# An attention and mixture-of-experts kernel on one core: order of x, maxima and first weights, and where sinks' rows and clearings are done

## The chip, the cores and the metric

One NeuronCore of a Trainium2 chip runs the whole program. The metric is the device time of one execution in microseconds. The kernel before takes 1252.02 us, the median of three runs (1251.76, 1252.02, 1252.05).

## The reference

Three layers follow one another. The change touches the first of them and the loads of weights for the second.

```python
# attention: q, k, v are (2, 8, 768, 64), n_sink = 4, window = 128
scores = scale * np.matmul(q, k.transpose(0, 1, 3, 2))
keep = is_sink | in_window            # keys 0..3, or 0 <= query - key < 128
scores = np.where(keep, scores, -1000000000.0)
a = np.exp(scores - scores.max(-1)) ; a = a / (a.sum(-1) + 1e-09)
x = (a @ v), heads side by side       # 1536 x 512
# SoLU layer: w_in (512, 1024), w_out (1024, 512)
h = x @ w_in ; solu = h * softmax(h) ; x = layernorm(solu) * g_ln @ w_out
# eight experts, every token through each
P = exp(x @ w_gate - max), 8 rounds of scaling rows and columns
out = sum over e of P[:, e] * (relu(x @ w1[e]) @ w2[e])
```

## The kernel before, in words

**Stages.** The program is written engine by engine; each engine runs its own list in order, and semaphores join them. The attention stage takes the first 93.88 us, then comes the SoLU layer (`h1_half` and what follows), then the experts. Where a product needs more than fp32r gives, both of its factors are split into a rounded part and a rest, and three products are summed (L797 to L799). So x, w_in, w_out and the sinks' rows of v each exist as a rounded part ("round_", "hi") and a rest ("rest_"), made by different instructions.

**Attention.** `PAIRS` is 8: a pair is two heads, side by side on the partitions (64 rows each). A head has `QT` = 6 tiles of 128 queries. A tile of queries sees its own 128 keys, the 128 before, and the 4 sinks, so its scores are 128, 256 or 260 columns wide. The probabilities at the sinks are handled apart, as `sink_cols`, since the rows of v at the sinks (`v_sink`, 72 partitions: a rounded copy at row 0, a second at row 32, the rest at row 64, each with 4 rows for either head) meet all tiles in one product.

**TensorE** goes through a pair as scores(p,1), back(p,0), scores(p,2), back(p,1), and so on up to scores(p+1,0), back(p,5). Scores (L722) lie in four banks, so the product for a tile waits until VectorE and ScalarE have read the one two tiles earlier. `back` does the rest of older tiles, three batches of two tiles to a pair: back(p,0) transposes batch 1 of pair p-1 (L742), back(p,1) multiplies its batch 0 by v (L766), back(p,2) transposes batch 2, back(p,3) transposes `sink_cols` (L750) and multiplies batch 1, back(p,4) transposes batch 0 of pair p itself, back(p,5) multiplies batch 2 and the sinks' rows (L773), which completes x of pair p-1. The first scores of a pair wait for its q and k (`qk_loaded`).

**VectorE** takes each tile from its bank, adds the mask and finds the row maximum in one instruction (`mask_max`, L1270). Between tiles its `back` normalises a batch (sum and reciprocal, L1278 and L1282, then the probabilities of one head, L1285), makes the rest of x (`rest_x`, L1303), copies transposed probabilities to SBUF (`copy_pT`, L1291) and makes the rest of v's sink rows (`rest_v_sinks`, L1297).

**ScalarE** takes the exponentials of each tile (L1042), scales probabilities (L1057), copies transposed ones (L1049, L1061) and rounds x of a pair (`round_x`, L1066), which frees the bank of x for the next pair together with `rest_x`.

**GpSimd** clears tensors and builds the masks (L481 to L509), and then in each pair: `normalise(p,0)` for the other head (L517), `rest_w_in` (L565), `normalise(p,1)`, `lay_sinks(p+1)` (L550: copies the sinks' columns of k beside each block), `rest_w_out` (L571), `normalise(p,2)`, `split_sinks` (L540, L543), `round_v_sinks` (L527), `round_segments(p+1)` (L556, L559). The weights of the SoLU layer come in eight segments, one for a pair, each 128x512 of w_in and of w_out, all through one buffer, `w_raw`. In pair 0 the order differs: normalise(0,0), normalise(0,1), lay_sinks(1), round_segments(0), rest_w_in(0), rest_w_out(0), normalise(0,2), and on.

**SyncE** issues all loads, in the order of its list. After q, k of pairs 0 and 1 it waits for the cleared `v_sink`, loads v of pair 0 (L400) with six little transfers of 4x64 into `v_sink` (L403), segment 0 (L408, L409), two small tensors and v of pair 1. Then comes the loop, whose order is: q and k of pair p, v of pair p-1, then segment p as soon as the rests of segment p-1 are made:

```python
for p in range(1, PAIRS):
    if p >= 2:
        sp.wait_ge(scores_full, STEPS * (p - 1))
        load_qk(p)
    if p >= 3:
        sp.wait_ge(x_full, p - 2)
        for h in range(2): load_v(p - 1, h)
    sp.wait_ge(in_done, p)      # rest_w_in(p - 1) is made
    sp.wait_ge(out_done, p)     # rest_w_out(p - 1) is made
    load_segments(p)
```

So q and k of pair 2 are issued behind segment 1, and this behind `rest_w_out(0)` (L571).

## Time and profile before

| | before |
|---|---|
| median of 3 runs | 1252.02 us |
| profiled execution | 1253.09 us |
| its span in the trace | 1251.3 us |
| TensorE busy | 1236.2 us, 99% |
| VectorE busy | 691.7 us, 55% |
| GpSimd busy | 535.7 us, 43% |
| ScalarE busy | 365.1 us, 29% |
| TensorE's share of the chain that ended last | 95% |

The span is the time from the first to the last instruction that the profiler recorded; the execution's own time is 1.8 us longer. Busy shares are means over the whole span, so they say little of the first 94 us, in which all four engines work side by side; a window over that stage alone has to be read for it. Timelines give the start of each instruction, its length, and in brackets the idle time of its engine before it with the work that ended it.

### The profile page before, as it was taken

How to read it: one execution, taken by the hardware profiler on the slowest of the kernel's cores; microseconds unless marked ns; L12 is line 12 of the kernel's file. 1: busy time of each engine (PE TensorE's matmuls, PEld its weight loads, DVE VectorE, ACT ScalarE, POOL GpSimd, SP SyncE). 2: the span in 40 equal slices, each digit the busy share in tenths (PEclk: the TensorE clock that was granted, in tenths of full speed). 3: DMA queues.
4: the chain of work that ended last, by engine and by line, in shares of the span. 5: the costliest groups of instructions: out<-in, count | busy, mean ns of one | idle time of the engine just before them, and what ended most of it. 6: DMA issues, size and time to landing. Idle time of an engine off the chain costs nothing.

```text
span 1251.3 us, 18785 instructions
## 1 busy us (share of the span) xinstructions
PE 1236.2 (99%) x6446; PEld 1097.3 (88%) x6446; DVE 691.7 (55%) x1348; ACT 365.1 (29%) x832; POOL 535.7 (43%) x625
## 2 busy tenths in 40 slices
PE   7999999999999999999999999999999999999998
PEld 4558899989988999999999999999999999999997
DVE  7895734356665555555555555555555555555554
ACT  7884634312233222222222222222222222222221
POOL 7772315644444444444444444444444444444440
PEclk9999999999999999999999999999999999999999
DMA  6440000111110111111111111111111111111102
GB/s 204 156 149 18 1 1 1 34 35 34 34 35 28 38 36 36 34 34 34 34 34 34 34 34 34 34 34 34 34 34 34 34 34 34 34 34 34 35 18 101
DMA packets 57264, 53.13 MB, mean 42 GB/s; under 512 B 4352, under 2 KB 44544, under 8 KB 57216
## 3 DMA queue, kind: packets, MB, share of 16 engines
q1 hardware_dynamic: 56928, 52.19, 13.1%
q8 instruction: 27, 0.44, 0.1%
q10 hardware_dynamic: 288, 0.33, 0.1%
q14 instruction: 21, 0.17, 0.0%
HBM read 49.35 MB, written 3.15 MB: 42 GB/s over the span
## 4 chain that ended last, share of the span: by engine, by line
PE 95%; ACT 2%; DVE 2%; DMA 1%; issue 1%; SPq 0%; DVEq 0%; ACTq 0%
PE ps L797 30%; PE ps L798 30%; PE ps L799 30%; PE ps L722 2%; PE ps L766 1%; PE ps L742 1%; PE ps L847 1%; ACT probs L1042 1%; ACT acc L1218 1%; DVE probs L1270 1%; DMA k_sb<-kT 0%; PE ps L977 0%; DVE xw L1303 0%; ACT xw L1066 0%; DMA q_sb<-qT 0%
## 5 line engine op out<-in xcount | busy, mean ns | idle before, releaser
L1528 DVE SCALAR_TENSOR_TENSOR acc<-ps,gate_now,acc 128x512 f32<-128x512 f32 x336 | 252.1, 750 | 166.2 <-PE ps L799 162.0
L797 PE MATMUL ps<-ring 128*128 128x512 f32 x768 | 300.6, 391 | 0.0
L798 PE MATMUL ps<-ring 128*128 128x512 f32 x768 | 299.8, 390 | 0.0
L799 PE MATMUL ps<-ring 128*128 128x512 f32 x768 | 299.2, 390 | 0.0
L1200 ACT ACTIVATE sums<-ps 128x384 f32<-128x384 f32 x192 | 94.4, 492 | 597.8 <-PE ps L799 597.8
L1504 DVE TENSOR_TENSOR sums<-ps,sums 128x384 f32<-128x384 f32 x192 | 106.9, 557 | 158.2 <-ACT sums L1200 106.9
L799 PEld LDWEIGHTS ps<-ring 128*128 128x128 f32 x768 | 144.3, 188 | 30.9
L797 PEld LDWEIGHTS ps<-ring 128*128 128x128 f32 x768 | 144.2, 188 | 27.9 <-DVE acc L1524 0.4
L798 PEld LDWEIGHTS ps<-ring 128*128 128x128 f32 x768 | 144.2, 188 | 25.8
L642 POOL TENSOR_TENSOR w_raw<-w_raw 128x256 f32<-128x256 f32 x32 | 23.7, 741 | 321.3 <-PE ps L799 321.3
L797 PE MATMUL ps<-xw,ring 128*128 128x384 f32 x448 | 152.5, 340 | 0.3 <-ACT sums L1200 0.2
L1510 DVE SCALAR_TENSOR_TENSOR ring<-sums,ring 128x384 fp32r<-128x384 f32 x192 | 112.0, 583 | 72.9 <-ACT ring L1211 72.9
L799 PE MATMUL ps<-xw,ring 128*128 128x384 f32 x448 | 151.0, 337 | 0.0
L798 PE MATMUL ps<-xw,ring 128*128 128x384 f32 x448 | 150.9, 337 | 0.0
L797 PE MATMUL ps<-xw,w_b 128*128 128x384 f32 x448 | 150.5, 336 | 0.0
L799 PE MATMUL ps<-xw,w_b 128*128 128x384 f32 x448 | 150.3, 336 | 0.0
L798 PE MATMUL ps<-xw,w_b 128*128 128x384 f32 x448 | 150.0, 335 | 0.0
L671 POOL TENSOR_SCALAR ring<-w_in 128x1024 fp32r<-128x1024 f32 x32 | 33.8, 1056 | 233.0 <-PE ps L799 178.2
L1211 ACT ACTIVATE ring<-sums 128x384 fp32r<-128x384 f32 x192 | 100.1, 521 | 85.7 <-DVE sums L1504 85.7
L797 PEld LDWEIGHTS ps<-xw,ring 128*128 128x128 f32 x448 | 84.1, 188 | 2.6 <-ACT sums L1200 0.5
L798 PEld LDWEIGHTS ps<-xw,w_b 128*128 128x128 f32 x448 | 84.3, 188 | 2.0
L797 PEld LDWEIGHTS ps<-xw,w_b 128*128 128x128 f32 x448 | 84.1, 188 | 1.9
(148 smaller groups left out, 1765.2 us busy)
## 6 DMA issues: line engine op xcount, KB each, us to landing
w_in<-w_exp SPq DMA_DIRECT2D x64, 256.0 KB, 3.2
w_raw<-w_exp SPq DMA_DIRECT2D x64, 128.0 KB, 2.8
w_raw<-w_exp SPq DMA_DIRECT2D x32, 256.0 KB, 3.2
v_sb<-v SPq DMA_DIRECT2D x16, 192.0 KB
out<-acc SPq DMA_DIRECT2D x12, 256.0 KB, 2.0
q_sb<-qT SPq DMA_DIRECT2D x7, 384.0 KB, 4.4
k_sb<-kT SPq DMA_DIRECT2D x7, 384.0 KB, 4.9
k_sb<-kT SPq DMA_DIRECT2D x9, 256.0 KB, 5.7
```

Of the source, the lines that this page charges most:

```text
L642: pool.tensor_tensor(raw(4), raw(0), raw(3), ALU.add).then_inc(w1_sums, 1)
L671: pool.tensor_scalar(w2c(0, 0, 2 * BANK), w2_raw(0, 2 * BANK), 1.0, 0.0, ALU.mult, ALU.add).then_inc(w2_hi, 1)
L722: pe.matmul(bank(k % S_BANKS)[:, 0:w], q_sb[rows_h, p % 2, t * P:(t + 1) * P], k_sb[rows_h, p % 2, k_at(t), at:at + w], start=True, stop=T ...
L742: last = pe.transpose(t_bank(p, use)[:, at:at + P], p_block(p, h, n), ident[:, :])
L797: pe.matmul(o, ws[0], xs[0], start=first, stop=False, skip_group_check=True)
L798: pe.matmul(o, ws[0], xs[1], start=False, stop=False, skip_group_check=True)
L799: return pe.matmul(o, ws[1], xs[0], start=False, stop=last, skip_group_check=True)
L1200: act.activation(part_sum(m, s), a_bank(s), ACT.Copy).then_inc(part_copied, 1)
L1211: act.activation(h_at(0, i, b * BLK, BLK), a_bank(s) if m == C12 else c_sum(m), ACT.Relu).then_inc(h_hi_out, 1)
L1504: dve.tensor_tensor(c_sum(m), at, part_sum(part, s), ALU.add).then_inc(c_summed, 1)
L1510: dve.scalar_tensor_tensor(out=h_at(1, i, b * BLK, BLK), in0=a_bank(s) if m == C12 else c_sum(m), scalar=0.0, in1=h_at(0, i, b * BLK, BLK) ...
L1528: dve.scalar_tensor_tensor(out=acc[:, T, :], in0=y_bank(u, T), scalar=gate_now[:, T:T + 1], in1=acc[:, T, :], op0=ALU.mult, op1=ALU.add).t ...
```

## The change

It has four parts, all in the attention stage.

1. **x first, maxima ahead.** On ScalarE `round_x(p-2)` stands ahead of the exponentials of pair p's first tile, and `scale_probs(p-1, 2)` moves from tile 0 to tile 1. On VectorE what stood between the masks of tile 0 and tile 1 (normalise(p-1,2), rest_x, copy_pT) now stands behind the masks of tile 1, with rest_x as the first of it.
2. **Sinks' rows of v in four parts.** All pairs' rows are loaded at the start by six transfers of 4x8x64, issued behind segment 0, in place of 48 of 4x64. GpSimd makes the rounded part and the rest for two pairs at once, in pairs 0, 2, 4 and 6; VectorE's L1297 is gone.
3. **Clearing by VectorE.** `v_sink` (now 72x1024), `sink_cols`, `wg` and `ones` are cleared or set by VectorE ahead of its first work, no longer by GpSimd.
4. **First weights.** In pair 0 GpSimd runs normalise(0,0), round_segments(0), normalise(0,1), lay_sinks(1), rest_w_in(0), normalise(0,2), split_sinks(0), rest_w_out(0), split_v_sinks(0), round_segments(1).

```diff
@@ sync
             def load_v(p, h):
                 sp.dma_start(v_sb[:, p % 2, h, :], v[p, h]).then_inc(v_loaded[p % 2], 16)
+            def load_v_sinks(h):
                 for row in (0, 32, 64):
                     row += h * NS
-                    sp.dma_start(v_sink[row:row + NS, p % 2, h * DH:(h + 1) * DH],
-                                 v[p, h, 0:NS, 0:DH]).then_inc(v_loaded[p % 2], 16)
+                    sp.dma_start(v_sink[row:row + NS, :, h * DH:(h + 1) * DH],
+                                 v[:, h, 0:NS, 0:DH].rearrange("p n d -> n p d")).then_inc(v_sinks_loaded, 16)
...
             load_qk(1)
-            sp.wait_ge(consts, 2)
             for h in range(2):
                 load_v(0, h)
             load_segments(0)
+            sp.wait_ge(v_sinks_clear, 1)
+            for h in range(2):
+                load_v_sinks(h)
...
@@ gpsimd
-            pool.memset(v_sink[:, :], 0.0).then_inc(consts, 1)
...
-            pool.memset(sink_cols[:, :, :].bitcast(F32), 0.0).then_inc(sinks_hi, 1)
...
-            pool.memset(ones[:, :], 1.0).then_inc(consts, 1)
-            pool.memset(wg[:, :, :].bitcast(F32), 0.0).then_inc(consts, 1)
...
+            def split_v_sinks(p):
+                two = slice(p, p + 2)
...
+                pool.tensor_scalar(v_sink_r[:, two, :], v_sink[:, two, :], 1.0, 0.0,
                                    ALU.mult, ALU.add).then_inc(v_sinks_hi, 1)
...
+                low = v_sink_r[64:SINK_ROWS, two, :]
+                pool.tensor_tensor(low, v_sink[64:SINK_ROWS, two, :], low.bitcast(F32),
+                                   ALU.subtract).then_inc(v_sinks_split, 1)
...
             for p in range(PAIRS):
                 normalise(p, 0)
-                if p > 0:
+                if p == 0:
+                    round_segments(0)
+                else:
                     rest_w_in(p)
                 normalise(p, 1)
                 if p + 1 < PAIRS:
                     lay_sinks(p + 1)
                 if p == 0:
-                    round_segments(0)
                     rest_w_in(0)
-                rest_w_out(p)
+                else:
+                    rest_w_out(p)
                 if p == 4:
                     rest_router()
                 normalise(p, 2)
                 split_sinks(p)
-                round_v_sinks(p)
+                if p == 0:
+                    rest_w_out(0)
+                if p % 2 == 0:
+                    split_v_sinks(p)
                 if p + 1 < PAIRS:
                     round_segments(p + 1)
@@ scalar
-                if t == 0 and p > 1:
-                    round_x(p - 2)
                 if t == 0 and p > 0:
                     copy_pT(p - 1, 1, 0)
+                if t == 1 and p > 0:
                     scale_probs(p - 1, 2)
...
             for p in range(PAIRS):
+                if p > 1:
+                    round_x(p - 2)
                 for t in range(QT):
@@ vector
-                if t == 0 and p > 0:
-                    normalise(p - 1, 2)
+                if t == 1 and p > 0:
                     if p > 1:
                         rest_x(p - 2)
+                    normalise(p - 1, 2)
                     copy_pT(p - 1, 1, 1)
...
-                if t == 3 and p > 0:
-                    rest_v_sinks(p - 1)
...
+            dve.memset(v_sink[:, :, :], 0.0).then_inc(v_sinks_clear, 1)
+            dve.memset(sink_cols[:, :, :].bitcast(F32), 0.0).then_inc(sink_cols_clear, 1)
+            dve.memset(wg[:, :, :].bitcast(F32), 0.0).then_inc(router_clear, 1)
+            dve.memset(ones[:, :], 1.0).then_inc(ones_set, 1)
```

GpSimd's list in pair 0, before:

```order
L517 TENSOR_TENSOR probs<-probs,a_stat 128x256
L517 TENSOR_TENSOR probs<-probs,a_stat 128x260 x2
L550 TENSOR_SCALAR k_sb<-k_sb 128x5x4 x2
L556 TENSOR_SCALAR xw<-w_raw 128x512
L559 TENSOR_SCALAR w_end<-w_raw 128x512
L565 TENSOR_TENSOR xw<-w_raw,xw 128x512
L571 TENSOR_TENSOR w_end<-w_raw,w_end 128x512
L517 TENSOR_TENSOR probs<-probs,a_stat 128x260 x2
L540 TENSOR_SCALAR sink_cols<-probs 128x4x8 x2
L543 TENSOR_TENSOR sink_cols<-probs,sink_cols 128x4x8
L527 TENSOR_SCALAR v_sink_r<-v_sink 72x128
```

and in the changed kernel, where lines are numbered anew (normalise L519, roundings L564 and L567, lay_sinks L558, rests L573 and L579):

```order
L519 TENSOR_TENSOR probs<-probs,a_stat 128x256
L564 TENSOR_SCALAR xw<-w_raw 128x512
L567 TENSOR_SCALAR w_end<-w_raw 128x512
L519 TENSOR_TENSOR probs<-probs,a_stat 128x260 x2
L558 TENSOR_SCALAR k_sb<-k_sb 128x5x4 x2
L573 TENSOR_TENSOR xw<-w_raw,xw 128x512
L519 TENSOR_TENSOR probs<-probs,a_stat 128x260 x2
L548 TENSOR_SCALAR sink_cols<-probs 128x4x8 x2
L551 TENSOR_TENSOR sink_cols<-probs,sink_cols 128x4x8
L579 TENSOR_TENSOR w_end<-w_raw,w_end 128x512
L528 TENSOR_SCALAR v_sink_r<-v_sink 72x256
L532 TENSOR_TENSOR v_sink_r<-v_sink,v_sink_r 8x256
```

Both roundings moved ahead of normalise(0,1), and the last instruction that SyncE's loop waits for (L571, now L579) moved behind normalise(0,2) and split_sinks.

VectorE's list where pair 1 passes into pair 2, before:

```order
L1270 ISA probs,a_stat<-ps,mask 128x128
L1270 ISA a_stat 128x1
L1278 TENSOR_SCALAR a_stat<-a_stat 128x4
L1282 RECIPROCAL a_stat<-a_stat 128x4
L1285 TENSOR_SCALAR probs<-probs,a_stat 128x260
L1303 TENSOR_TENSOR xw<-ps,xw 128x768
L1291 COPY pT<-ps 128x512
L1270 ISA probs,a_stat<-ps,mask 128x256
L1270 ISA a_stat 128x1
```

and in the changed kernel (masks L1287, normalise L1295 to L1302, copy L1308, rest_x L1314):

```order
L1287 ISA probs,a_stat<-ps,mask 128x128
L1287 ISA a_stat 128x1
L1287 ISA probs,a_stat<-ps,mask 128x256
L1287 ISA a_stat 128x1
L1287 ISA probs,a_stat<-ps,mask 128x256
L1287 ISA a_stat 128x1
L1314 TENSOR_TENSOR xw<-ps,xw 128x768
L1295 TENSOR_SCALAR a_stat<-a_stat 128x4
L1299 RECIPROCAL a_stat<-a_stat 128x4
L1302 TENSOR_SCALAR probs<-probs,a_stat 128x260
L1308 COPY pT<-ps 128x512
```

The masks of both heads of tile 1 (128x256) moved ahead of the other four steps, and rest_x ahead of normalise.

SyncE's list from the loads of v of pair 0 on, before:

```order
L400 DMA v_sb<-v 128x384
L403 DMA v_sink<-v 4x64 x3
L400 DMA v_sb<-v 128x384
L403 DMA v_sink<-v 4x64 x3
L408 DMA w_raw<-w_in 128x512
L409 DMA w_raw<-w_out 128x512
```

and in the changed kernel:

```order
L402 DMA v_sb<-v 128x384 x2
L412 DMA w_raw<-w_in 128x512
L413 DMA w_raw<-w_out 128x512
L407 DMA v_sink<-v 4x8x64 x6
L427 DMA g_col<-g_ln 128x8
L428 DMA wg_raw<-w_gate 128x32
```

The segment is now issued ahead of all transfers to `v_sink`; the loop behind it keeps its order.

## Rows read from the trace of the kernel before

**Rows 1.** Windows: length, busy us of PE, PEld, DVE, ACT, POOL, clock, DMA share, GB/s.

```profile
3.00:11.00 8.00, 6.89 (x34) 4.77 (x34) 5.76 (x29) 5.60 (x22) 4.41 (x13) 1.00 1.06 359
23.70:80.65 56.95, 53.58 (x395) 33.71 (x395) 50.72 (x187) 48.21 (x159) 42.30 (x83) 1.00 0.53 175
93.88:1251.30 1157.42, 1153.95 (x5863) 1045.34 (x5863) 612.31 (x1049) 288.71 (x583) 465.73 (x483) 1.00 0.10 32
```

**Rows 2.** Timeline of TensorE at pair 2: start, length, what, idle before it.

```profile
23.72 0.49 PE L722 MATMUL ps<-k_sb,q_sb 64*128 64x128 f32 x4 [1.27 <-DMA k_sb<-kT]
```

**Rows 3.** Timeline of the DMA queue of SyncE: start, issue time.

```profile
7.19 0.35 SPq L408 DMA_DIRECT2D w_raw<-w_in  x1
...
15.56 0.35 SPq L408 DMA_DIRECT2D w_raw<-w_in  x1
```

**Rows 4.** Chain of waits, pair 2: start, length.

```profile
17.95 5.72 DMA k_sb<-kT
```

**Rows 5.** DMA issues up to 9 us: count, size, us to landing.

```profile
w_raw<-w_in SPq DMA_DIRECT2D x1, 256.0 KB, 4.0
```

**Rows 6.** Issue times in ns of one DMA line: minimum/median/maximum.

```profile
L409 SPq DMA_DIRECT2D w_raw<-w_out x3: 432/433/892, 7.6 to 26.3; - x3
```

**Rows 7.** Timeline of GpSimd in pair 0.

```profile
10.25 1.25 POOL L517 TENSOR_TENSOR probs<-probs,a_stat 128x260 f32<-128x260 f32 x2 [1.22 <-DVE a_stat L1282]
11.47 0.38 POOL L550 TENSOR_SCALAR k_sb<-k_sb 128x20 f32<-128x20 f32 x2
...
12.97 1.27 POOL L565 TENSOR_TENSOR xw<-w_raw,xw 128x512 fp32r<-128x512 f32 x1
14.20 1.27 POOL L571 TENSOR_TENSOR w_end<-w_raw,w_end 128x512 fp32r<-128x512 f32 x1
15.43 1.25 POOL L517 TENSOR_TENSOR probs<-probs,a_stat 128x260 f32<-128x260 f32 x2
16.87 0.40 POOL L540 TENSOR_SCALAR sink_cols<-probs 128x32 fp32r<-128x32 f32 x2 [0.19 <-POOL probs L517]
...
17.57 0.30 POOL L527 TENSOR_SCALAR v_sink_r<-v_sink 72x128 fp32r<-72x128 f32 x1
```

**Rows 8.** Timeline of VectorE at the start and in pair 1.

```profile
3.96 0.56 DVE L1328 COPY k_sb<-k_sb 128x20 f32<-128x20 f32 x2 [3.11 <-DMA q_sb<-qT]
...
21.57 0.42 DVE L1285 TENSOR_SCALAR probs<-probs,a_stat 128x260 f32<-128x260 f32 x1
```

**Rows 9.** Timeline of VectorE, pair 4 (begun at 46.19).

```profile
48.69 0.17 DVE L1278 TENSOR_SCALAR a_stat<-a_stat 128x4 f32<-128x4 f32 x1 [0.40 <-ACT probs L1042]
...
49.11 0.82 DVE L1285 TENSOR_SCALAR probs<-probs,a_stat 128x260 f32<-128x260 f32 x1
50.15 0.96 DVE L1303 TENSOR_TENSOR xw<-ps,xw 128x768 fp32r<-128x768 f32 x1 [0.23 <-ACT xw L1066]
51.03 0.68 DVE L1291 COPY pT<-ps 128x512 f32<-128x512 f32 x1
51.62 0.41 DVE L1270 CUSTOM_DVE_ANT_0 probs<-ps,mask 128x256 f32<-128x256 f32 x1
...
55.62 0.50 DVE L1297 TENSOR_TENSOR v_sink_r<-v_sink,v_sink_r 8x128 fp32r<-8x128 f32 x1
```

**Rows 10.** Timeline of GpSimd, pair 4.

```profile
49.15 1.25 POOL L517 TENSOR_TENSOR probs<-probs,a_stat 128x260 f32<-128x260 f32 x2 [0.38 <-DVE a_stat L1282]
```

**Rows 11.** Timeline of ScalarE, pair 4.

```profile
52.08 0.51 ACT L1042 ACTIVATE probs<-probs,a_stat 128x256 f32<-128x256 f32 x1 [1.08 <-DVE a_stat L1270]
...
54.07 0.57 ACT L1049 ACTIVATE pT<-ps 128x512 f32<-128x512 f32 x1
```

**Rows 12.** Timeline of TensorE, pairs 4 and 5.

```profile
54.79 0.60 PE L750 MATMUL ps<-ident,sink_cols 128*72 128x128 f32 x4
...
57.57 0.49 PE L722 MATMUL ps<-k_sb,q_sb 64*128 64x128 f32 x4
...
59.66 0.70 PE L722 MATMUL ps<-k_sb,q_sb 64*128 64x256 f32 x4
```

More of the change, by code:

```diff
@@ L121, in solu_moe @@
         SINK_ROWS = 64 + 2 * NS
-        v_sink = sb("v_sink", [SINK_ROWS, 2, P], F32, in_a)
-        v_sink_r = sb("v_sink_r", [SINK_ROWS, 2, P], F32R, in_a)
+        v_sink = sb("v_sink", [SINK_ROWS, PAIRS, P], F32, in_a)
+        v_sink_r = sb("v_sink_r", [SINK_ROWS, PAIRS, P], F32R, in_a)
         sink_cols = sb("sink_cols", [P, QT - 2, SINK_ROWS], F32R, in_a)
@@ L219, in solu_moe @@
         sinks_hi, sinks_split = sem("sinks_hi"), sem("sinks_split")
+        sink_cols_clear, router_clear, ones_set = sem("sink_cols_clear"), sem("router_clear"), sem("ones_set")
+        v_sinks_clear, v_sinks_loaded = sem("v_sinks_clear"), sem("v_sinks_loaded")
         v_sinks_hi, v_sinks_split = sem("v_sinks_hi"), sem("v_sinks_split")
@@ L519, in normalise @@
                 last.then_inc(probs_ready[1], 1)
-            def round_v_sinks(p):
-                pool.wait_ge(v_loaded[p % 2], 128 * (p // 2 + 1))
-                if p >= 2:
-                    pool.wait_ge(x_full, p - 1)
+            def split_v_sinks(p):
+                two = slice(p, p + 2)
                 if p == 0:
-                    pool.wait_ge(consts, 2)
-                pool.tensor_scalar(v_sink_r[:, p % 2, :], v_sink[:, p % 2, :], 1.0, 0.0,
+                    pool.wait_ge(v_sinks_loaded, 96)
+                pool.tensor_scalar(v_sink_r[:, two, :], v_sink[:, two, :], 1.0, 0.0,
                                    ALU.mult, ALU.add).then_inc(v_sinks_hi, 1)
+                pool.wait_ge(v_sinks_hi, p // 2 + 1)
+                low = v_sink_r[64:SINK_ROWS, two, :]
+                pool.tensor_tensor(low, v_sink[64:SINK_ROWS, two, :], low.bitcast(F32),
+                                   ALU.subtract).then_inc(v_sinks_split, 1)
+                pool.wait_ge(v_sinks_split, p // 2 + 1)
             def split_sinks(p):
@@ L534, in split_sinks @@
                     pool.wait_ge(probs_ready[h], BATCHES * (p + 1))
-                if p > 0:
+                if p == 0:
+                    pool.wait_ge(sink_cols_clear, 1)
+                else:
                     pool.wait_ge(pT_full, T_USES * (p - 1) + SINK_USE + 1)
@@ L541, in split_sinks @@
                 last.then_inc(sinks_hi, 1)
-                pool.wait_ge(sinks_hi, p + 2)
+                pool.wait_ge(sinks_hi, p + 1)
                 pool.tensor_tensor(sink_cols[:, :, 32:32 + n], a, sink_cols[:, :, 0:n].bitcast(F32),
@@ L581, in _ @@
                 normalise(p, 0)
-                if p > 0:
+                if p == 0:
+                    round_segments(0)
+                else:
                     rest_w_in(p)
@@ L587, in _ @@
                 if p == 0:
-                    round_segments(0)
                     rest_w_in(0)
-                rest_w_out(p)
+                else:
+                    rest_w_out(p)
                 if p == 4:
@@ L594, in _ @@
                 split_sinks(p)
-                round_v_sinks(p)
+                if p == 0:
+                    rest_w_out(0)
+                if p % 2 == 0:
+                    split_v_sinks(p)
                 if p + 1 < PAIRS:
@@ L758, in pv @@
                 if b == 0:
-                    pe.wait_ge(v_loaded[p % 2], 128 * (p // 2 + 1))
+                    pe.wait_ge(v_loaded[p % 2], 32 * (p // 2 + 1))
                     if p > 0:
@@ L771, in pv_sinks @@
                 pe.wait_ge(*copied(p, SINK_USE))
-                pe.wait_ge(v_sinks_split, p + 1)
-                pe.matmul(x_psum(2, QT), v_sink_r[:, p % 2, :], sinkT[:, :],
+                pe.wait_ge(v_sinks_split, p // 2 + 1)
+                pe.matmul(x_psum(2, QT), v_sink_r[:, p, :], sinkT[:, :],
                           start=False, stop=True, skip_group_check=True).then_inc(x_full, 1)
@@ L788, in back @@
                     if p == 0:
-                        pe.wait_ge(consts, 3)
+                        pe.wait_ge(consts, 2)
                     turn(p, 0)
@@ L990, in gate_step @@
                 if step == "logits":
+                    pe.wait_ge(ones_set, 1)
                     gate_logits()
@@ L1091, in _ @@
                     act.wait_ge(small_loaded, 32)
-                    act.wait_ge(consts, 5)
+                    act.wait_ge(router_clear, 1)
                     act.activation(wg[:, :, WG_AT:WG_AT + EXPERTS], wg_raw[:, :, :], ACT.Copy).then_inc(wg_ready, 1)
@@ L1155, in tile @@
                 turned_pair(T + 1, 1)
+            round_x(PAIRS - 2)
             back(PAIRS, 0)
+            back(PAIRS, 1)
             exp_h(0)
@@ L1335, in _ @@
                     back(p, t)
-            back(PAIRS, 0)
+            back(PAIRS, 1)
             TURNED = {4: (0, 0), 5: (0, 4), 7: (1, 0), 8: (1, 4), 10: (2, 0), 11: (2, 4)}
@@ L1403, in _ @@
             copy_pT(PAIRS - 1, 2, 1)
-            rest_v_sinks(PAIRS - 1)
             solu(1)
```

7 lines of the change are left out of this document (1 added, 6 removed).

## Prediction

> **What bounds the kernel now.** I read the windows first, because the change touches only the attention stage. From 93.88 us to the end TensorE is busy 1153.95 of 1157.42 us, at the full clock (1.00), and VectorE and GpSimd are busy for about half and two fifths of it [rows 1]. Nothing there waits for what the change moves, so that stretch keeps its length, and whatever the attention stage gains or loses goes to the end one for one. The stage before it is 93.88 us, 7.5% of the kernel.
>
> Inside it the windows show a different picture. From 23.70 to 80.65 us five pairs of heads pass, 56.95 us or 11.39 us for each; PE is busy 53.58 us, DVE 50.72, ACT 48.21 and POOL 42.30 [rows 1]. No engine is full, so a loop of waits through several engines sets the period. The timelines of pair 4 give its steps [rows 9 to 12].
>
> The start is bound by something else. The timeline of TensorE shows that the scores of pair 2 began at 23.72 us after 1.27 us of idleness that a load of k ended [rows 2], and the chain of waits goes through that same load, issued at 17.95 and 5.72 us long [rows 4]. Its issue is late because SyncE's queue runs in order: the weights of the next segment are issued ahead of it, at 15.56 [rows 3], and they wait until GpSimd has finished the rest of the first w_out segment (L571), which ended when the next instruction began, at 15.43 [rows 7].
>
> **The change part by part.**
>
> *First weights, another order on GpSimd.* Before, pair 0 ran: normalise(0,1), lay_sinks, two roundings, rest_w_in, rest_w_out, normalise(0,2), split_sinks. Now the roundings stand ahead of normalise(0,1), and rest_w_out stands behind split_sinks. Two things follow.
>
> First, the roundings wait for the weights. These were issued at 7.19 us [rows 3] and landed 4.0 us later [rows 5], at 11.2. They are now issued sooner, since the six little v transfers that stood ahead come behind them, but from 3 to 11 us the DMA share was 1.06 [rows 1]: the engines were full of q, k and v loads, so I leave the landing at 11.2. GpSimd was free to begin normalise(0,1) at 10.25 [rows 7]; now it stands behind the wait.
>
> Second, the end of rest_w_out moves. From the timeline of GpSimd [rows 7]: normalise took 11.47 - 10.25 = 1.22 us, lay_sinks and both roundings 12.97 - 11.47 = 1.50, rest_w_in 1.23, rest_w_out 1.23, normalise(0,2) with split_sinks 17.57 - 15.43 = 2.14. The new order from the landing: 11.2 + 1.22 + 1.50 + 1.23 + 2.14 + 1.23 = 18.5 us, where 15.43 stood. SyncE's queue, which waits for exactly this, is **3.1 us later**: the weights of segment 1, and behind them q and k of pair 2. From the issue of the weights to the landing of k it took 17.95 + 5.72 - 15.56 = 8.1 us. Within it one issue took 0.89 us where the median of its line is 0.43 [rows 6], so 7.6 is possible. k for pair 2 then lands between 18.6 + 7.6 = 26.2 and 18.65 + 8.1 = 26.8, against 23.7: TensorE was 1.27 us idle there already, so all of it counts. I take **+2.8 us**, bounds +2.5 and +3.1. The pieces of work that are moved cost the same; what costs is that a queue stands behind the last one.
>
> *x first, and the maxima of tile 1 ahead.* On ScalarE round_x of the pair before last stands ahead of the exponentials of tile 0. On VectorE the masks of tile 1 (L1270) come before rest_x (L1303), and normalise(p-1,2) behind it. Before, VectorE idled 0.40 us for exponentials and 0.23 for round_x [rows 9], and ScalarE 1.08 us for the masks of tile 1 [rows 11]. These waits go, and the loop closes elsewhere: TensorE issues scores(p,1) behind the last products with v, so the masks of tile 1 wait for it. I add the new loop once round. TensorE from the transposed sinks to the scores of the next pair, 57.57 - 54.79 = 2.78; on to scores of tile 1, 59.66 - 57.57 = 2.09; until these are complete 0.70 [rows 12]. VectorE: two masks, 0.41 each less the 0.07 by which neighbours overlap, 0.69; rest_x, 51.03 - 50.15 = 0.88; normalise, 49.11 - 48.69 = 0.42 and 0.82 less 0.08, 1.16; copy, 0.59 [rows 9]. Then the mask of tile 2 to its exponential, 52.08 - 51.62 = 0.46 [rows 9, 11]; two exponentials, half of 54.07 - 52.08, 1.00; the copy that frees the bank and TensorE's start behind it, 54.79 - 54.07 = 0.72 [rows 11, 12]. Sum 11.07 us, against 11.39: 0.32 less per pair. Over five pairs and the last interval up to 93.88 that is 1.9 us. It is a sum without chance holds, which the measured 11.39 contains, and so I count half: **-1.0 us**, bounds 0 and -1.9.
>
> One step of this sum rests on a hold. VectorE's L1285 took 0.82 us in pair 4 and 0.42 in pair 1 [rows 8, 9]; in pair 4 GpSimd had begun its own normalise 0.04 us after it [rows 10] and VectorE ended well behind GpSimd's first instruction. The same two are released together in the new order, so 0.82 stays in my sum. The Trainium skill (SBUF — State Buffer, section Who interferes with whom) says that whoever issues first of a two-port VectorE instruction and a GpSimd one gets the shared pair of ports for the whole instruction. By that rule VectorE, which began first, would not have been held. The row differs, and the row decides; by the rule the period would be some 0.4 shorter, which is in a rival below.
>
> *Sinks' rows of v, in four parts.* 48 little DMAs become 6, and 16 small operations (L527, L1297) become 8, all on GpSimd in pairs 0, 2, 4 and 6. VectorE loses L1297, 0.50 us in pair 4 [rows 9]; on the new loop it doesn't stand, since it came between masks of tile 3 and 4, so I count nothing twice. GpSimd gets two instructions in even pairs; the old rounding was 0.30 for 128 columns [rows 7], twice the columns and a difference are 0.5 to 1.2 us. They are hidden: POOL is busy 42.30 of 56.95 us [rows 1]. In pair 0 they stand behind rest_w_out, and ahead of roundings that wait for weights anyway. If that cover were gone, normalise(1,0) would be up to 1.2 us later; the late k load behind it still covers that.
>
> *Clearing by VectorE.* Four memsets of 1024 + 288 + 896 + 128 = 2336 columns. The nearest row is rest_x, 768 columns in 0.88 us [rows 9], so some 2.7 us. VectorE idled 3.11 us before 3.96, for q [rows 8]. Hidden, cost 0; if each column took a third more, 0.6 us of the start, which the wait for the weights until 11.2 covers. GpSimd's masks come earlier, and nobody waits for them.
>
> **Sum.** +2.8 - 1.0 = +1.8 us. The profiled execution took 1253.09 us (span 1251.3), which gives 1254.9 for one like it; it lies 1.07 over the median of the runs, 1252.02, so against the median I forecast **1253.8 us**, or 0.14% more. A measurement of this kernel can tell about 0.2%, 2.5 us, from no change.
>
> **The rivals.**
>
> *Slower, 1255.1.* The late k load comes in full (+3.1) and the period does not shorten, because the loop through scores(p,1), masks, rest_x, normalise is held as often as the old one. For it: VectorE's three steps now stand in one row behind a single release by TensorE, and two of the three can be held by GpSimd. Against it: the sum of the rows. It decides if the period stays at 11.3 or more. 1252.02 + 3.1 = 1255.1. Chance 0.35, with what is worse.
>
> *Faster, 1249.4.* TensorE becomes the bound. Its busy time is 53.58 / 5 = 10.72 us per pair; at that period six intervals give back 6 x 0.67 = 4.0 us. The roundings start sooner too, if the weights, now issued earlier, land 1.2 us earlier, when GpSimd is free at 10.25 or before: the loss is then about 1.4. Net -2.6, 1249.4. A period that short needs, among other things, the hold of 0.4 us to go, as by the skill's rule above. Against it stand the row of 0.82, the DMA share of 1.06 and the sum of 11.07. It decides if the period falls under 10.8. Chance 0.1.
>
> *Nothing to be told, 1252.6.* Loss and gain are nearly equal: the loss at its lower bound 2.5 and the gain at its full 1.9. Chance 0.2; the forecast itself, 1253.8, has 0.35.
>
> **How the numbers follow.** Limits of 0.2% are 1249.5 and 1254.5. Faster than that: the second rival, 0.1. Slower: the first rival, 0.35. Between them: forecast and near-cancelling, 0.55. The range goes from 1250.8 (half way between the near-cancelling case and the fast rival) to 1255.8 (the slow rival and 0.1 us more for each of seven pairs).
>
> **What would show it.** In the changed profile, the weights of segment 1 should be issued at about 18.6 us and not 15.56, the scores of pair 2 should start at 26.2 to 26.9 behind an idle time of 3 us or more ended by k, GpSimd should wait about 2 us for weights ahead of the first rounding, and scores should follow from pair to pair at 11.1 to 11.3 us, with VectorE idle about 1 us before the masks of tile 1, for TensorE. The first product of the next stage should start 1 to 3 us after 93.88. The forecast is wrong if the scores of pair 2 start before 25 us (then the queue was not what held them), or if the period is under 10.8 or over 11.5.

## The result, and the profile after

| | before | changed |
|---|---|---|
| median, six runs each | 1252.19 us | 1256.54 us (1255.23 to 1258.77) |
| ratio | | 1.0035, interval 1.0023 to 1.0046 |
| profiled execution | 1253.09 us | 1258.03 us |
| its span | 1251.3 us | 1256.2 us |
| first product of the next stage | 93.88 us | 98.92 us |

The change made the kernel 4.35 us slower. The sign is that of the forecast; the time is 2.7 us over its 1253.8 and 0.7 us outside my range. The windows of the changed kernel (length, busy us of PE, PEld, DVE, ACT, POOL, clock, DMA share, GB/s) stand against [rows 1]:

```profile
3.00:11.00 8.00, 6.84 (x34) 4.77 (x34) 5.86 (x33) 5.69 (x23) 2.33 (x9) 1.00 1.06 356
20.70:26.05 5.35, 0.58 (x5) 0.32 (x4) 1.25 (x5) 1.97 (x8) 4.36 (x7) 0.91 0.80 268
26.05:40.55 14.50, 14.50 (x79) 8.56 (x80) 8.44 (x32) 8.39 (x27) 7.67 (x16) 0.68 0.38 136
40.55:74.25 33.70, 31.20 (x238) 19.44 (x237) 28.25 (x112) 29.79 (x101) 25.47 (x50) 1.00 0.54 177
98.92:1256.20 1157.28, 1153.87 (x5864) 1045.30 (x5863) 612.15 (x1048) 288.36 (x582) 465.95 (x483) 1.00 0.10 32
```

The last stretch is as long as before (1157.28 against 1157.42 us), so the attention stage holds all of it, as forecast. Three pairs at full clock take 33.70 us, 11.23 each. What no step of mine had is the third row: pair 2 takes 14.50 us, TensorE is busy all the time, and the granted clock is 0.68 on average. Microsecond by microsecond:

```profile
24.00:25.00 1.00, 0.46 (x3) 0.23 (x3) 0.50 (x2) 0.00 (x0) 1.00 (x1) 1.00 1.05 369
25.00:26.00 1.00, 0.00 (x0) 0.00 (x0) 0.75 (x5) 0.56 (x3) 1.00 (x3) 0.52 0.18 56
...
34.00:35.00 1.00, 1.00 (x8) 0.57 (x8) 1.00 (x5) 0.11 (x1) 0.75 (x3) 0.50 0.68 245
35.00:36.00 1.00, 1.00 (x10) 0.50 (x6) 0.93 (x5) 0.99 (x4) 0.92 (x3) 0.86 0.04 16
```

The clock falls to its lower level, 1.2 in place of 2.4 GHz, at 25 us and comes back at 35. The Trainium skill (TensorE: Matmul & The Clock Gate, Part 1) says that this gate is set by how busy the engine has been of late. For the fall the trace agrees, since an almost idle stretch lies ahead of it. The rise came only after TensorE had worked without a pause for 9.2 us, from 26.05 us on. TensorE's timeline shows what went ahead of it, against [rows 2]:

```profile
20.18 0.55 PE L755 MATMUL ps<-ident,probs 128*128 128x128 f32 x3
23.92 0.55 PE L755 MATMUL ps<-ident,probs 128*128 128x128 f32 x3 [3.19 <-POOL probs L519]
26.05 0.80 PE L735 MATMUL ps<-k_sb,q_sb 64*128 64x128 f32 x4 [1.58 <-DMA k_sb<-kT]
26.77 2.40 PE L779 MATMUL ps<-pT,v_sb 128*64 128x256 f32 x12
29.11 0.80 PE L786 MATMUL ps<-sinkT,v_sink_r 72*128 72x512 f32 x1
```

Between 20.7 and 26.05 us TensorE did three transposes (0.58 us). It waited first for GpSimd's normalise(1,0), then for k; then four score products took 0.80 us where 0.49 is usual [rows 2]. Why GpSimd was late is on its timeline, against [rows 7]:

```profile
10.95 0.62 POOL L564 TENSOR_SCALAR xw<-w_raw 128x512 fp32r<-128x512 f32 x1 [2.02 <-DMA w_raw<-w_in]
...
17.51 1.28 POOL L579 TENSOR_TENSOR w_end<-w_raw,w_end 128x512 fp32r<-128x512 f32 x1
18.75 0.41 POOL L528 TENSOR_SCALAR v_sink_r<-v_sink 72x256 fp32r<-72x256 f32 x1
19.25 0.72 POOL L532 TENSOR_TENSOR v_sink_r<-v_sink,v_sink_r 8x256 fp32r<-8x256 f32 x1
21.69 0.62 POOL L564 TENSOR_SCALAR xw<-w_raw 128x512 fp32r<-128x512 f32 x1 [1.72 <-DMA w_raw<-w_in]
22.31 0.62 POOL L567 TENSOR_SCALAR w_end<-w_raw 128x512 fp32r<-128x512 f32 x1
22.89 0.97 POOL L519 TENSOR_TENSOR probs<-probs,a_stat 128x128 f32<-128x128 f32 x2
```

L579 ends at 18.8, SyncE issues the weights at 18.88 (the queue's rows below, against [rows 3]), they land at 21.6, two roundings follow, and only then normalise(1,0), which TensorE needs. The late queue thus held TensorE twice: through the weights and through k.

```profile
5.12 0.56 SPq L412 DMA_DIRECT2D w_raw<-w_in  x1
...
18.88 0.33 SPq L412 DMA_DIRECT2D w_raw<-w_in  x1
...
20.80 0.61 SPq L398 DMA_DIRECT2D k_sb<-kT  x1
```

**The account of the profiled execution.** Scores of pair 2 start at 26.05 and not 23.72: +2.33. From there to the scores of pair 3 it takes 14.50 us and not 10.56 (34.28 - 23.72): +3.94. From the scores of pair 3 to the next stage 58.37 (98.92 - 40.55) and not 59.60: -1.23. Together +5.04.

### The profile page after: what moved, and what is told of

Read it like the earlier page. It is cut to its first block, busy times and chain, and to the rows that moved or that the text cites. A ratio compares the mean times of both kernels' runs of the same rounds, so it can differ in the third digit from the quotient of the medians.

```text
span 1256.2 us, 18733 instructions
## 1 busy us (share of the span) xinstructions
PE 1237.9 (99%) x6446; PEld 1097.5 (87%) x6446; DVE 685.9 (55%) x1344; ACT 364.7 (29%) x832; POOL 534.8 (43%) x621
## 4 chain that ended last, share of the span: by engine, by line
PE 94%; DMA 1%; ACT 1%; DVE 1%; issue 1%; SPq 1%; POOL 1%; DVEq 0%; ACTq 0%; POOLq 0%
PE ps L810 30%; PE ps L811 30%; PE ps L812 30%; PE ps L779 1%; PE ps L735 1%; DMA k_sb<-kT 1%; PE ps L860 1%; PE ps L755 1%; ACT acc L1235 1%; DMA w_raw<-w_out 0%; PE ps L990 0%; ACT probs L1056 0%; PE ps L786 0%; DVE xw L1314 0%; PE ps L763 0%
```

## The experiments

All ratios are to the kernel before, run beside on the same chip. Its own median was between 1252.25 and 1253.10 us in these groups, so differences below about 1 us between kernels of different groups tell nothing, and ratios whose intervals overlap are not told apart.

**e1: the changed kernel with GpSimd's order of pair 0 as before.** In `for p in range(PAIRS)` of GpSimd:

```diff
-                if p == 0:
-                    round_segments(0)
-                else:
+                if p > 0:
                     rest_w_in(p)
                 normalise(p, 1)
...
                 if p == 0:
+                    round_segments(0)
                     rest_w_in(0)
-                else:
-                    rest_w_out(p)
+                rest_w_out(p)
...
-                if p == 0:
-                    rest_w_out(0)
```

> The changed kernel with GpSimd's order of pair 0 as before; all else stays changed. Theory (clock): the new order makes the load of k for pair 2 2.4 us late, and the longer idleness of TensorE lets the granted clock fall to half of full speed from about 25 to 35 us, which costs some 3 us more. Then here k lands at 23.7, the clock stays at 1.00 throughout, scores follow at 11.23 us, the first product of the next stage starts between 92.5 and 93.7 us, and the time is 0.3 to 1.5 us under the kernel before. Rival (x first): the order on ScalarE and VectorE disturbs pair 2 and brings the half clock; then the clock still falls here and the time is 3 us or more over the kernel before. Rival (clearing or v's sink rows): the same, with GpSimd late in pair 0.

1251.79 us, ratio 0.9987 (0.9979 to 0.9996). Scores of pair 2 at 23.70, clock 1.00, next stage at 92.93. The order of the first weights is the cause of the loss: without it the kernel is 1.3 us under the one before by the medians, with it 4.4 over (e13), 5.7 us for this one part. One of the eleven runs of e1 (1253.88 us) has a mean clock of 0.997, so a low clock can occur without the new order too.

**e2: that order alone, in the kernel before** (the same edit the other way).

> The kernel before with only GpSimd's new order of pair 0. Theory (clock): k for pair 2 lands at 26 to 26.8 us, the granted clock falls to 0.5 at about 25 us and comes back at about 35, the first product of the next stage starts near 99.5 us, and the time is 4.5 to 6 us over the kernel before. Rival (only the delay): the clock stays at 1.00 and the time is 2.4 to 3.1 us over. Rival (the parts only cost together): under 1 us over.

1257.77 us, ratio 1.0033 (1.0023 to 1.0042; the profiled execution 1255.87). TensorE idle for 3.13 us, the clock falls inside this idleness and comes back at 29:

```profile
22.00:23.00 1.00, 0.00 (x0) 0.00 (x0) 0.00 (x0) 0.00 (x0) 1.00 (x3) 0.78 1.03 364
23.00:24.00 1.00, 0.56 (x3) 0.50 (x3) 0.00 (x0) 0.00 (x0) 1.00 (x2) 0.50 0.99 344
...
29.00:30.00 1.00, 1.00 (x6) 0.64 (x7) 0.18 (x1) 0.79 (x1) 0.00 (x0) 0.81 1.04 387
```

The three of its twelve runs with a mean clock of 0.999 or 1.000 took 1254.57 to 1255.51 us, the nine at 0.996 or 0.997 took 1255.87 to 1260.41. The loss is 4.7 us by the medians and 4.1 by the ratio, on the theory's side; the next stage (96.81) came earlier than I had put it, with 7 and not 10 us at the low clock.

**e3: the order of x and maxima alone, in the kernel before.** ScalarE's and VectorE's part of the diff.

> The kernel before with only the order of x and maxima on ScalarE and VectorE. Theory: the period of the pairs 3 to 6 is 11.23 us and not 11.39 or more, nothing else moves, the clock stays at 1.00, time 0.3 to 1.5 us under the kernel before. Rival: the order costs in pair 2, where TensorE comes out of a wait; then scores(3) start after 34.9 us and the time is as before or over it.

1282.34 us, ratio 1.0227: both theories missed by far. From pair 2 on, scores follow at 15.6 to 16.9 us, and VectorE's timeline shows where:

```profile
30.65 0.29 DVE L1285 TENSOR_SCALAR probs<-probs,a_stat 128x128 f32<-128x128 f32 x1
```

is the shortest normalising instruction in the kernel before, and in e3:

```profile
66.08 3.53 DVE L1288 TENSOR_SCALAR probs<-probs,a_stat 128x128 f32<-128x128 f32 x1
```

GpSimd's timeline beside it:

```profile
65.91 0.30 POOL L527 TENSOR_SCALAR v_sink_r<-v_sink 72x128 fp32r<-72x128 f32 x1
66.18 0.62 POOL L556 TENSOR_SCALAR xw<-w_raw 128x512 fp32r<-128x512 f32 x1
66.76 0.62 POOL L559 TENSOR_SCALAR w_end<-w_raw 128x512 fp32r<-128x512 f32 x1
67.34 0.97 POOL L517 TENSOR_TENSOR probs<-probs,a_stat 128x128 f32<-128x128 f32 x2
68.27 1.26 POOL L565 TENSOR_TENSOR xw<-w_raw,xw 128x512 fp32r<-128x512 f32 x1
```

VectorE's instruction began 0.17 us after GpSimd's L527 and ended at 69.61, when GpSimd's row, without a gap, had ended at 69.53. It happens in each pair from pair 2 on, pairs counted from 0 (3.40 or 3.53 us), and the clock falls behind it (0.81 on average from 40.15 to 56.69 us). The Trainium skill (SBUF — State Buffer, section Who interferes with whom) says that the engine that issues second is fully blocked from the shared ports while the first one's instruction runs; the rows agree on who waits, but the wait here lasted over six instructions of the other engine.

**e9: parts 2 and 3 alone** (sinks' rows of v in four parts, clearing by VectorE), the changed kernel with parts 1 and 4 undone.

> The kernel before with the sinks' rows of v in four parts and the clearing by VectorE, and nothing else. My reading: hidden work, time within 1 us of the kernel before, period of the pairs 11.4 to 11.5 us, no half clock. Rival: GpSimd's two instructions ahead of the rounding of segment 1 make k or the weights late, 1 us or more over the kernel before. Rival: VectorE's saving shortens the period to 11.2 us without the order of x; then the order of x is worth nothing.

1250.21 us, ratio 0.9978 (0.9969 to 0.9987): 2.5 us faster, at least all that the change gains in e1, from parts that I had priced at nothing. The last rival came true: VectorE's saving shortens the pairs, and more than I had given it, to 11.05 us without the order of x. Scores of pair 2 start as before (23.74 us, before 23.72), so the gain lies behind them, and the clearing, which ends at the start, has no part in it. Part 2 took L1297 from VectorE, and also instructions from GpSimd and small transfers; which of these shortens the pairs was not tested apart. Odd and even pairs take the same 11.05 us, though GpSimd has its new instructions in the even ones only, which speaks for L1297. VectorE by lines, 30 to 94 us of the kernel before:

```profile
L1297 DVE TENSOR_TENSOR v_sink_r<-v_sink,v_sink_r 8x128 fp32r<-8x128 f32 x6 | 3.7, 610 | 0.2
```

**e11: e3, with round_v_sinks behind round_segments on GpSimd.**

> e3 (x first alone, 1282 us), with GpSimd's rounding of v's sink rows (L527) behind the rounding of the next segment and not ahead of it. In e3 VectorE's 128x128 instruction of normalise(p,0) began while L527 ran and took 3.53 us in place of 0.29, until GpSimd had ended its row of five instructions. Theory (a hold that depends on which GpSimd instruction is running when VectorE's begins): moved so that another one runs, the 3.53 us are gone in all pairs, and the time is 1251 to 1253 us. Rival (the hold comes from the order of x, with any GpSimd instruction): the 3.5 us stay, 1275 us or more.

1256.31 us, ratio 1.0030 (1.0019 to 1.0042). The 3.53 us are gone (0.39), so the hold doesn't come with the order of x as such; it hangs on what GpSimd runs around the start of VectorE's instruction. Whether that is the kind of instruction or the moment isn't told apart. But another is held, which the change had removed:

```profile
45.86 1.75 DVE L1300 TENSOR_TENSOR v_sink_r<-v_sink,v_sink_r 8x128 fp32r<-8x128 f32 x1
```

It ends at 47.61, GpSimd's L565 at 47.46. The order of x without part 2 is a loss in both placings of round_v_sinks, 3.6 and 29 us.

**e4, e5, e14: TensorE kept busy.** The changed kernel with products of `ident` by `ident` in its idle time; e4 has 20 and 8 of them, e5 12 and 5, e14 10 and 3.

```diff
                     last.then_inc(pT_full, 1)
+                    if p == 1 and b == 0 and h == 0:
+                        for _ in range(12):
+                            pe.matmul(ps[:, 6 * BANK:6 * BANK + P], ident[:, :], ident[:, :],
+                                      start=True, stop=True, skip_group_check=True)
...
+                        if p == 1:
+                            for _ in range(5):
+                                pe.matmul(ps[:, 6 * BANK:6 * BANK + P], ident[:, :], ident[:, :],
+                                          start=True, stop=True, skip_group_check=True)
                         scores(p + 1, 0)
```

> The changed kernel, with 20 products of ident by ident (128x128, fp32) in TensorE's idle time between the transposes of the two heads of batch 1 of pair 1, and 8 more ahead of the scores of pair 2; they write a part of PSUM that nobody reads. k is as late as in the changed kernel. Theory (clock): the granted clock stays at 1.00 all the time, scores(2) still start at 26.0 to 26.5, scores(3) at 36.4 to 37.5 and not at 40.55, and the time is 2.8 to 4 us under the changed kernel, 0.5 to 1.6 over the kernel before. Rival (queues): pair 2 is long because GpSimd and the weights of segment 2 are late behind the wait, whatever the clock; then scores(3) start after 39 us here too and the time is that of the changed kernel.

> As e4, with 12 and 5 filling products in place of 20 and 8, so that they end before the scores of pair 2 have their k. Theory (clock): the granted clock stays at 1.00, scores(2) start at 26 to 26.5 us unless the weights land late as in e4, scores(3) 11.2 to 11.5 us later, the next stage at 95.3 to 96.3, and the time is 1 to 2.5 us over the kernel before (ratio 1.001 to 1.002), the lateness of k less the shorter period. Rival: the delay alone is worth all of the loss; then the ratio is again 1.0035.

> As e5 with 10 and 3 fillers. In e4 the fillers outlasted the wait by 1.2 us, and e5's profile had a start 2.3 us late. Theory (the half clock costs about 3 us): the fillers end ahead of k, the clock stays at 1.00, scores(3) follow scores(2) by 11.2 us and not 14.5, and the median is 2 to 3.5 us under e13. Rival (the half clock costs TensorE time that it would have waited anyway): median within 1 us of e13.

```profile
28.02:39.25 11.23, 10.39 (x80) 6.47 (x80) 8.47 (x32) 8.14 (x27) 7.25 (x15) 1.00 0.55 176
```

In e4 (this window) and e5 the clock stays at 1.00 and pair 2 takes 11.23 us, so the low clock cost 14.50 - 11.23 = 3.3 us in the profile of the changed kernel. In e14 TensorE was still idle for 1.68 us behind the fillers, the clock fell, and pair 2 took 12.81. The medians didn't follow: 1256.75, 1256.54 and 1256.70, ratios 1.0027, 1.0036, 1.0035, which are the numbers of the rivals of e5 and e14. In e4 both w_out of segment 1 and the fillers made the scores of pair 2 late (28.02), the fillers ending 1.2 us after k had landed; in e5 the profiled execution was late from its start (scores of pair 1 at 12.62). These name a delay for one execution each, and not for the median.

**e13: the changed kernel again, beside e14 and e15.**

> The changed kernel once more, beside e14 and e15 on one chip: 1.0035 of the kernel before, with a mean clock of 0.996 to 0.999.

1256.75 us, 1.0035 (1.0022 to 1.0047). Its profiled execution (1258.57) is as slow as the first one's, and put together otherwise:

```profile
7.84 3.49 PE L735 MATMUL ps<-k_sb,q_sb 64*128 64x260 f32 x12 [1.03 <-DMA k_sb<-kT]
11.27 1.54 PE L755 MATMUL ps<-ident,probs 128*128 128x128 f32 x6
...
27.42 0.83 PE L755 MATMUL ps<-ident,probs 128*128 128x128 f32 x3 [3.89 <-POOL probs L519]
28.47 0.80 PE L735 MATMUL ps<-k_sb,q_sb 64*128 64x128 f32 x4 [0.22 <-DMA k_sb<-kT]
```

Here TensorE waited 1.03 us for k of pair 0, and until 17 us everything ran at half rate: six transposes in 1.54 us, where the changed kernel's first trace has

```profile
9.49 0.87 PE L755 MATMUL ps<-ident,probs 128*128 128x128 f32 x6
```

The granted clock reads 1.00 in both. So scores of pair 2 start at 28.47, but the low clock lasts only from 27.5 to 31 us, and pair 2 takes 12.38 us.

**e6, e15, e16, e17: k ahead of the weights, without and with fillers.** e6 issues q and k of pair 2 ahead of the loop; e15 adds 10 fillers in the first wait; e16 and e17 are two more traces of e15.

```diff
+            sp.wait_ge(scores_full, STEPS)
+            load_qk(2)
             for p in range(1, PAIRS):
-                if p >= 2:
+                if p >= 3:
```

> The changed kernel with q and k of pair 2 issued on SyncE ahead of the weights of segment 1. k is then there by 18 us. Theory: TensorE's other wait remains, 3 us for GpSimd's normalise(1,0), which stands behind two roundings that wait for the weights of segment 1; scores(2) start at 24 to 25 us. If that idleness alone brings the half clock (in e2 the clock fell at 22.8 us, inside it), the time is 2 to 4 us over the kernel before; if the wait for k is needed for the fall, the clock stays at 1.00 and the time is within 0.7 us of the kernel before.

> As e6 (k ahead of the weights; one idleness of 3.04 us, for GpSimd's normalise(1,0); clock at 0.996 to 1.00 in its runs, median 1.0019 of the kernel before) with 10 fillers in that idleness. Theory: clock 1.00 in every run, scores(3) 11.2 us behind scores(2) and not 13.39, median 1.0005 of the kernel before or less. Rival: the same 1.002 as e6.

> The kernel of e15 once more, for its trace. In e15 the profiled execution was the fastest (1252.74 us, clock 0.999), the median 1255.59 with clocks of 0.999 to 1.000. If a slow execution is one with a late start, the trace shows TensorE idle 0.6 to 1.1 us for k of pair 0 near 7.5 us, then six transposes in 1.54 us in place of 0.87 until about 16 us, and scores(1) at 12.2 to 12.8 us in place of 10.3; scores(3) still follow scores(2) by 11.2 us. If the slow executions have the early start, something else costs their 3 us, behind the fillers.

> As e16, a third trace: over 1254.5 us goes with scores(1) behind 12 us, under 1253.5 us with scores(1) at 10.4 us.

e6: 1254.86 us, 1.0019 (1.0010 to 1.0028). No wait for k, 3.04 us for GpSimd, and the clock still falls, at 25 us (pair 2 in 13.39 us): the wait through the weights is enough.

```profile
23.58 0.55 PE L757 MATMUL ps<-ident,probs 128*128 128x128 f32 x3 [3.04 <-POOL probs L521]
25.00:26.00 1.00, 1.00 (x10) 0.62 (x6) 0.83 (x8) 0.90 (x3) 1.00 (x3) 0.51 0.00 0
```

In e6 the four runs with a mean clock of 0.999 or 1.000 took 1252.95 to 1254.27 us, the seven at 0.996 or 0.997 took 1254.61 to 1256.59, so here as in e2 every run with a low clock is slower than every run without; but these may also have waited longer, and so this is no price of the clock alone. e15: median 1255.59, 1.0027, no better. Its three traces differ: 1252.74 us has the early start and pair 2 in 11.23, though the clock was low for 3.4 us in pair 1, ahead of the fillers; 1254.22 the half rate until 16 us (scores of pair 1 at 11.64, pair 2 in 11.59); 1255.71 the early start, but w_out of segment 1 landed 1.3 us after the rounding of w_in, TensorE was idle for 2.43 us behind the fillers, and pair 2 took 12.82. My expectation for e17 (over 1254.5 us with scores of pair 1 behind 12 us) was thus wrong: a start at half rate, weights that land late and the low clock each appear in one of these executions and not in another, and fillers of a fixed count stand against the last alone, and in e17 not even that. The low clock of the fastest:

```profile
14.00:15.00 1.00, 1.00 (x6) 0.67 (x6) 0.98 (x1) 1.00 (x5) 1.00 (x2) 0.52 1.01 356
15.00:16.00 1.00, 1.00 (x6) 0.34 (x6) 1.00 (x2) 0.12 (x1) 1.00 (x3) 0.50 0.46 162
```

What the low clock makes of the median, apart from the other two, stays open; in the traces pair 2 is 1.2 to 3.3 us longer with it (12.38 to 14.50 against 11.23).

**e7, e10: the new order of pair 0 with nothing queued behind it.** e7 is e6 with segment 1 rounded behind normalise(1,0) on GpSimd; e10 has q and k of every later pair ahead of the weights too.

```diff
-                if p == 0:
-                    round_segments(0)
-                else:
-                    rest_w_in(p)
+                if p < 2:
+                    round_segments(p)
+                if p > 0:
+                    rest_w_in(p)
...
-                if p + 1 < PAIRS:
+                if 0 < p and p + 1 < PAIRS:
                     round_segments(p + 1)
```

> As e6, and GpSimd rounds segment 1 behind normalise(1,0) and not ahead of it. Theory: neither k nor weights hold TensorE, idle time between 20 and 26 us is under 1 us, no half clock, scores(2) at 21.5 to 22.7 us; gain against the kernel before 1.5 to 3 us (about 1250). Rival: the new order of pair 0 costs elsewhere, by late weights of segment 2 or a late k of pair 3; then the time is that of the kernel before.

> The changed kernel (GpSimd's new order of pair 0 kept) with q and k of every pair from 2 on issued ahead of the weights, and segment 1 rounded behind normalise(1,0): e8 with the new order. Theory: the new order costs only through what waits behind it on SyncE's queue; with k taken out of that queue it equals e8, within 0.7 us (1248.5 to 1250). Rival: the late weights of segments 1 and 2 hold GpSimd and with it the pair; then it stands at 1251 to 1252 like e7.

e7: 1251.99 us, 1.0000 (0.9991 to 1.0009); TensorE's waits ahead of scores(2) are gone (21.33 us), but it waits 0.81 us for k of pair 3, and the gain is away. e10: 1250.55, 0.9983 (0.9974 to 0.9992). Against e6, e7 has only the rounding of segment 1 moved, and is 2.9 us faster by the medians, 2.4 by the ratios: so much at least the wait through the weights, with its low clock, costs when k is on time. With k out of the queue too (e10) the order as such costs about 1.1 us against e8 by the ratios (0.9983 and 0.9974).

**e8, e12, e18: the best of the parts.** e8 is e1 with both edits (for all pairs, below); e12 is e9 with both; e18 is e8, where SyncE waits for k of pair 0 before it issues v.

```diff
             for p in range(1, PAIRS):
-                if p >= 2:
-                    sp.wait_ge(scores_full, STEPS * (p - 1))
-                    load_qk(p)
                 if p >= 3:
...
                         load_v(p - 1, h)
+                if p + 1 < PAIRS:
+                    sp.wait_ge(scores_full, STEPS * p)
+                    load_qk(p + 1)
                 sp.wait_ge(in_done, p)
```

> As e1 (the changed kernel with GpSimd's order of pair 0 as before), with q and k of every pair from 2 on issued ahead of the segment's weights, and segment 1 rounded behind normalise(1,0). Theory: TensorE waits for no k at all (0.22 and 0.16 us in e1), scores(2) at 21.5 to 22.7 us, gain 1 to 2 us over e1, which makes 1249.5 to 1250.5. Rival: k was no longer the last wait in e1, and VectorE's or GpSimd's work holds pair 2; then it equals e1.

> e9 (sinks' rows and clearing alone, 11.05 us per pair) with q and k of every pair from 2 on issued ahead of the weights and segment 1 rounded behind normalise(1,0): e8 without the order of x. In e9 TensorE waited 1.77 us for k of pair 2, once. Theory: that wait goes, so 1 to 1.8 us less than e9, 1248.4 to 1249.2, ratio about 0.997 or below. Rival (only the end of a chain): a wait of VectorE or GpSimd behind the k takes its place, and it equals e9, 0.9978.

> e8 (the fastest so far, 1248.98 us, 0.9974), with SyncE waiting for the last k and q of pair 0 before it issues v and the first weights. Theory (the late start comes from transfers issued right behind k of pair 0): that k lands by 6.9 us in every execution, scores(1) at 10.3 us, and no run is over 1250 us; median 1248.7 to 1249.2. Rival (the landing of that k varies with what was issued ahead, q and k of pair 1): late starts stay, runs of 1251 to 1252 us among the others. Rival (the weights land too late): GpSimd waits for them, 1 us or more over e8 in all runs.

e8: **1248.98 us**, 0.9974 (0.9963 to 0.9984), the lowest median, 3.3 us under the kernel before; its interval overlaps that of e9. e12: 1250.58, 0.9987 (0.9978 to 0.9996), no better than e9: the 1.77 us wait for k is gone (22.06 us), and a wait takes its place in pair 2, so that scores of pair 3 come at 34.21, where e9 has 34.19:

```profile
27.91 0.87 PE L777 MATMUL ps<-pT,v_sb 128*64 128x256 f32 x8 [0.97 <-DVE xw L1309]
```

e8 and e12 differ only by the order of x, and here it is e8, with that order, that is 1.6 us faster by the medians. In the traces (that of e8 has the late start) e12 has the shorter pairs from pair 4 on (11.06 against 11.23 us) and the longer pairs 1 and 2 (11.69 and 12.15 against 11.26 and 11.23).

e18: 1249.29, 0.9977; five of its eleven runs took 1251.15 to 1252.66, and its trace has the longest wait for k of pair 0:

```profile
8.26 3.49 PE L734 MATMUL ps<-k_sb,q_sb 64*128 64x260 f32 x12 [1.50 <-DMA k_sb<-kT]
```

So v and weights behind that k are not what makes it late. What does stays open; q and k of pair 1, issued ahead, remain a candidate.

## Why the prediction was wrong

**The queue behind rest_w_out: right.** GpSimd's sum gave the end of L571 (now L579) at 18.5 us, it came at 18.8; weights issued "at about 18.6", measured 18.88; k at 26.2 to 26.8, measured 26.0; scores of pair 2 at "26.2 to 26.9", measured 26.05. Taken as +2.8 with a lower bound of +2.5, measured +2.33, a little under it. That the end of L579 fits so well is partly luck: w_in landed 0.25 us before my 11.2, and then w_out was waited for, 0.45 us, which my sum left out. e1 shows that the order is what moved the queue.

**The missing term: the low clock.** The step that failed is "TensorE was 1.27 us idle there already, so all of it counts. I take +2.8 us". I wrote down an idle time of 3 us or more and priced it at its length. Behind 5.35 us with 0.58 busy the granted clock went to the lower level for 10 us, 3.3 us more in the first profile. I had also not followed the second way in which the queue is late, through the weights to normalise(1,0), which stands behind the roundings of segment 1. Only of a delay by GpSimd's new instructions, up to 1.2 us, I wrote that "the late k load behind it still covers that". In length k does cover it: k landed last. But TensorE waited 3.19 us for normalise(1,0) and 1.58 for k, with half a microsecond of work between, and e6 shows that the first of these alone brings the low clock. The remaining 0.67 us of pair 2 (11.23 against 10.56) goes with the new order of x: pair 2 takes 11.47 us in e1 and 10.45 in e9. For the profiled execution this closes the account: +5.04 is 3.24 over my +1.8, the low clock is 3.3 of it, and the queue (0.5 less than I took) and the order of x (0.4 less gain) nearly cancel. For the median, 2.7 us over the forecast, the split isn't shown. There the runs show that the order of the first weights costs 5.7 us (e13 against e1) and about 1.1 once neither k nor normalise(1,0) stands behind the weights (e10 against e8), so that most of the loss comes through these two waits; how much of it is the waits' length and how much the clock stays open, since the fillers, which kept the clock up in e4 and e5, gained nothing in the median.

**x first: the size right by luck, the reason wrong.** "-1.0 us", half of what a loop of 11.07 us would give; measured 11.23 per pair, and in e1, with parts 1 to 3 only, 69.23 us from scores(2) to the next stage against 70.16. But e9 needs 67.52 for it without the order of x. The step that failed is that of the sinks' rows: "on the new loop it doesn't stand ... so I count nothing twice". L1297 stood between the masks on the old loop, 0.61 us on average, and part 2, which removed it, gave the gain without any order of x. What the order of x adds has no fixed sign: from e9 to e1 it takes 1.1 us back by the ratios (0.9978 and 0.9987, intervals that overlap; 1.7 us in the traces), from e12 to e8 it gives 1.6 us. I compared the new loop with the measured period of the kernel before, and so credited the difference to the first of two parts that both touched it. Alone the order of x costs 29 us (e3).

**The hold in that sum** (0.82 us stays) was right: L1302 takes 0.81 behind rest_x in every pair from 2 on of the changed kernel. That such a hold can last 3.5 us was in no rival.

**Late loads.** k of pair 7 was waited for, 0.56 us, which I had not looked for. **Clearing** is hidden, as forecast: four memsets end at 3.3 us, before k lands at 3.9.

**The range.** Its lower end was to be half way between 1252.6 and 1249.4, which is 1251.0 and not 1250.8; nothing hangs on it.

The nearest rival was "slower, 1255.1", with the right sign and the wrong mechanism: it let the period stay at 11.3 or more, and only pair 2 and the last interval, with its wait for k (74.25 to 86.12), were that long.

## What to carry to other kernels

Where a change makes an engine that was busy wait longer, price more than the wait: look at how much work is left in the whole stretch, and put the clock's fall, with the price from rows at the lower level, among the rivals. When an instruction is moved, follow everything that waits for it through every queue, and to each engine behind the queue, before the first number is written. When two parts touch the same loop, work out the loop with each of them alone; a gain that belongs to one can hide a loss of the other, and the order of x has one sign beside e9 and another beside e12.

## What the runs showed that I had not expected

A VectorE instruction of 0.29 us took 3.53 us beside a row of GpSimd instructions without a gap (e3), and 0.39 when one GpSimd instruction stood elsewhere (e11). At the start TensorE's work can run at half rate until 16 or 17 us with a granted clock of 1.00 in the records: e1, e5, e8, e13 and e18 show it behind a wait of 0.6 to 1.5 us for the last k of pair 0, e16 without such a wait; in e10 and e11 the wait is there and the half rate ends at about 12.5 us. These profiled executions are 1.4 to 3.5 us over the fastest of their kernels; what else differed in them isn't known. And the low clock lasted 3.4 and 10 us in two executions of the same program (e13 and the first trace). That alone doesn't order its times: the one with 3.4 us was the slower (1258.57 against 1258.03), with the start at half rate.
